# Attention, ELU layer and gated experts on one core: two large SBUF buffers are allocated after the small tensors instead of before them

## The reference

```python
q, k, v: [4, 8, 576, 64] float32        # window of 64 positions back
scores = q @ k.T / sqrt(64), masked to 0 <= i - j < 64
x = softmax(scores) @ v                 # reshaped to 2304 tokens x 512
h = x @ w_in                            # 512 -> 2048
x = where(h > 0, h, exp(min(h, 0)) - 1) @ w_out
P = exp(x @ w_gate - max)               # 2304 x 8, then 8 rounds of row and
for _ in range(8):                      # column normalisation
    P /= P.sum(1) + 1e-9; P /= P.sum(0) + 1e-9; P *= N / E
for e in range(8):                      # 512 -> 1024 -> 512 per expert
    out += P[:, e:e+1] * (relu(x @ w1[e]) @ w2[e])
```

## The kernel before

| tensor | start byte | size | start modulo 64 |
|---|---|---|---|
| `yacc` | 1,152 | 36,864 | 0 |
| `xs` | 38,016 | 24,576 | 0 |
| `w1t`, `w2t` | 62,592 and 91,264 | 28,672 each | 0 |
| `wraw` | 119,936 | 28,672 | 0 |
| `pb` | 148,608 | 9,216 | 0 |
| `scratch` | 157,824 | 67,584 | 0 |
| `ss` (over `scratch`) | 157,824 | 43,008 | 0 |
| `hb` (over `scratch`) | 200,832 | 24,576 | 0 |
| `ident`, `ones`, `wg` | 225,408; 225,920; 226,432 | 512 each | 0 |
| `adder` | 226,944 | 32 | 0 |
| `gate` | 226,976 | 576 | 32 |
| `token_max`, `all_max`, `gate_shift`, `row_sum` | 227,552 to 227,648 | 4, 4, 4, 72 | 32, 0, 32, 0 |
| `col_part`, `col_sum` | 227,744; 227,776 | 32 each | 32, 0 |
| `share` | 227,808 | 512 | 32 |
| `logit_parts` | 228,320 | 1,024 | 32 |

## Time and profile before

### The profile page before, as it was taken

One profiled execution on the slowest core, in us unless ns is written; L12 is line 12 of the kernel. 1 busy time (PEld: TensorE's weight loads), 2 busy tenths in 40 slices (PEclk: granted clock), 3 DMA queues, 4 the chain that ended last, 5 costly groups with the idle time before them and its releaser, 6 DMA issues.

```text
span 1897.3 us, 31366 instructions
## 1 busy us (share of the span) xinstructions
PE 1869.2 (99%) x11628; PEld 1834.2 (97%) x11628; DVE 1497.2 (79%) x1834; ACT 847.5 (45%) x1411; POOL 648.6 (34%) x513
## 2 busy tenths in 40 slices
PE   8989999999999999999999999999999999999998
PEld 6779999999999999999999999999999999999998
DVE  5767877878998888878778778787787787787877
ACT  6866655656664524333334243343333333432422
POOL 6733242333243343232332423332423324233220
PEclk9989999999999999999999999999999999999999
DMA  9974766663466666766666666667666666666654
GB/s 255 296 290 142 253 218 209 212 217 139 187 217 229 241 235 209 246 216 219 218 226 215 218 217 229 216 207 250 209 225 217 223 225 209 220 232 207 219 185 150
DMA packets 96653, 414.73 MB, mean 219 GB/s; under 512 B 9576, under 2 KB 10744, under 8 KB 96504
## 3 DMA queue, kind: packets, MB, share of 16 engines
q1 hardware_dynamic: 96504, 412.74, 63.5%
HBM read 374.88 MB, written 37.82 MB: 218 GB/s over the span
## 4 chain that ended last, share of the span: by engine, by line
PE 90%; DVE 4%; issue 2%; ACT 1%; POOL 1%; DMA 1%; SPq 0%; DVEq 0%; ACTq 0%; POOLq 0%
PE ps L1317 29%; PE ps L1312 29%; PE ps L1319 29%; PE ps L1276 1%; PE ps L1302 1%; PE ps L1292 1%; DVE hb L1052 1%; DVE xs L944 1%; DMA wraw<-moe_w_out_dram 1%; DVE yacc L1079 0%; DVE hb L1006 0%; DVE ss L978 0%; POOL scratch L566 0%; ACT pb L811 0%; ACT pb L816 0%
## 5 line engine op out<-in xcount | busy, mean ns | idle before, releaser
L799 ACT ACTIVATE ss<-hb 128x768 fp32r<-128x768 f32 x420 | 347.6, 843 | 595.3 <-DVE hb L1059 284.7
L1312 PE MATMUL ps<-xs,w1t 128*128 128x384 f32 x1680 | 564.3, 336 | 9.9 <-DMA xs<-x_store 2.7
L1312 PE MATMUL ps<-ss,w2t 128*128 128x384 f32 x1680 | 563.1, 335 | 3.1 <-DVE yacc L1079 3.1
L1317 PE MATMUL ps<-xs,w1t 128*128 128x384 f32 x1680 | 564.8, 336 | 0.0
L1319 PE MATMUL ps<-xs,w1t 128*128 128x384 f32 x1680 | 563.4, 335 | 0.0
L1317 PE MATMUL ps<-ss,w2t 128*128 128x384 f32 x1680 | 563.2, 335 | 0.0
L1319 PE MATMUL ps<-ss,w2t 128*128 128x384 f32 x1680 | 562.4, 335 | 0.0
L1079 DVE TENSOR_TENSOR yacc<-ps,yacc 128x768 f32<-128x768 f32 x396 | 377.8, 954 | 165.8 <-PE ps L1319 160.9
L978 DVE TENSOR_TENSOR ss<-hb,ss 128x768 fp32r<-128x768 f32 x420 | 400.5, 957 | 21.2 <-ACT ss L799 11.4
L595 POOL TENSOR_TENSOR w1t<-wraw,w1t 128x512 fp32r<-128x512 f32 x140 | 187.3, 1350 | 486.1 <-DVE ss L978 306.1
L595 POOL TENSOR_TENSOR w2t<-wraw,w2t 128x512 fp32r<-128x512 f32 x140 | 184.7, 1339 | 444.1 <-DVE hb L1001 226.9
(11 more groups left out here) (101 smaller groups left out, 1286.5 us busy)
## 6 DMA issues: line engine op xcount, KB each, us to landing
xs<-x_store SPq DMA_DIRECT2D x388, 768.0 KB, 4.3
wraw<-moe_w_dram SPq DMA_DIRECT2D x32, 1024.0 KB, 7.1
x_store<-xs SPq DMA_DIRECT2D x32, 768.0 KB, 3.6
pb<-p_store SPq DMA_DIRECT2D x24, 384.0 KB, 4.3
x_store<-w2t SPq DMA_DIRECT2D x10, 768.0 KB, 6.5
scratch<-q_dram SPq DMA_DIRECT2D x16, 288.0 KB, 5.3
scratch<-k_dram SPq DMA_DIRECT2D x16, 288.0 KB, 6.8
scratch<-v_dram SPq DMA_DIRECT2D x16, 288.0 KB, 7.8
```

Source lines behind the costliest of these rows:

```text
L799: nc.scalar.activation(ss[:, step, 0, :], hq(r, HOME[step]), ACT.Copy).then_inc(s_hi_done, 1)
L1312: nc.tensor.matmul(bank, w_parts[:, step, 0, cols], hi, start=step in FRESH and kt == 0, stop=False, skip_group_check=True)
L1317: nc.tensor.matmul(bank, w_parts[:, step, 0, cols], lo, start=False, stop=False, skip_group_check=True)
```

## The change

The block that allocates `scratch`, `ss` and `hb` is moved from before `ident` to after `logit_parts`. Nothing else differs: no instruction, wait, queue or tensor size.

```diff
         pb = sb("pb", [P, CHUNKS, CT])
-
-        SS = STEPS * 2 * QN
-        HB = 2 * 4 * QN
-        with nc.sbuf_tensor("scratch", [P, SS + HB], F32) as scratch_tensor:
-            scratch_space = scratch_tensor[:]
-        ss = sb("ss", [P, STEPS, 2, QN], F32R)
-        hb = sb("hb", [P, 2, 4, QN])
         ident = sb("ident", [P, P])
         ones = sb("ones", [P, P])
...
         p_turned = logit_parts[0:PT]
+
+        SS = STEPS * 2 * QN
+        HB = 2 * 4 * QN
+        with nc.sbuf_tensor("scratch", [P, SS + HB], F32) as scratch_tensor:
+            scratch_space = scratch_tensor[:]
+        ss = sb("ss", [P, STEPS, 2, QN], F32R)
+        hb = sb("hb", [P, 2, 4, QN])
```

## The result

The changed kernel is slower: median 1920.98 us (1918.61 to 1921.98, 4 runs) against 1897.83 us (1895.19 to 1899.97, 4 runs) before, ratio 1.012 with a 95% interval of 1.0103 to 1.0139. That is 23.15 us. The profiled execution took 1919.68 us.

A forecast was written before the change was run, and what follows sets the result against it. The prediction took TensorE's matmul rate as the bound. Its five prices, 0 + 0 + 0 + 0 + 0, left the profiled 1899.13 us, so it forecast 1899 us, range 1891 to 1908, with 0.78 for no change within 0.3%.

The forecast's parts named there:

- The bound: Whole kernel: TensorE's matmul rate, 10,080 x 0.173 = 1744 us of 1897; placement matters through that rate or lateness beyond cover.
- each ns on a matmul of the product down: Product down, L1312, L1317, L1319: each ns costs 5.04 us; 1.13 ns per matmul would exceed the 5.7 us no-change margin.
- Matmuls that read `ss`: Product down, 5,040 matmuls with ss at 32 modulo 64: price taken as 0, upper bound 36 us.
- The rival: Product down: moving reads of ss at 32 modulo 64 get dearer, with an extra 64-byte piece 1935 us; chance 0.07.
- VectorE, ScalarE and GpSimd at 32 modulo 64: Elementwise work and attention: at most 10 ns per VectorE instruction, 3 ns per ScalarE, GpSimd 0; all hidden, cost 0.
- The loads of attention: 64 q, k, v loads into scratch: taken as 0, upper 2.4 us; rival that they come late, 1905 us, chance 0.03.
- The granted clock from 110 to 155 us: Sign to check in the changed kernel's profile, from 110 to 155 us: the clock stays near 0.89.
- The estimate from the Trainium skill: Rows of q and k in scratch: 79 beats of 76 by the 256-byte rule, 4%, sum about 1 us longer.
- another phase at start-up: Rival, 110 to 155 us: other arrival times remove clock loss and a GpSimd wait, giving 1891.4 us; chance 0.09.

The follow-up runs named there:

- e2: Kernel before, with adder (32 bytes) allocated ahead of scratch, so scratch, ss and hb move by only 32 bytes; 1894.95 us.
- f4: Kernel before, with ident, ones, wg, share and logit_parts ahead of scratch, so ss and hb go up by 3,072 bytes; 1893.04 us.
- r2: The kernel with ss and hb 3,072 bytes up from the kernel before, timed in five rounds; 1895.82 us, ratio 0.9999.
- g1: Kernel before, with three 32-byte tensors ahead of w2t: w2t and ss 96 bytes later, xs and w1t stay; 1903.38 us.
- g2: Kernel before, with xs and ss moved by 96 bytes modulo 256 and both weights w1t and w2t by 0; 1924.58 us.
- f3: Kernel before, with all tensors 160 bytes lower, so their differences of place stay; 1900.91 us.
- e4: Kernel before, with adder between ss and hb: hb alone at 32 modulo 64, ss at 0; 1895.84 us.
- r1: Changed kernel, with adder, col_part and col_sum behind hb, so ss moves up 3,840 bytes instead of 3,936; 1895.66 us, ratio 0.9999.
- e1: Changed kernel, with adder (32 bytes) allocated behind hb, so ss and hb start at multiples of 64; 1902.78 us, ratio 1.0039.
- f1: Kernel before, with step s of ss 32 x s bytes later and all tensors 896 bytes lower; 1903.43 us.
- f2: Kernel before, with step s of ss 128 x s bytes later, 0 to 768; 1899.83 us.

## Why the prediction was wrong

**The bound was read rightly.** TensorE's rate of matmuls sets the time, and a change of placement moves it only through that rate. The statement that each ns on a matmul of the product down costs 5 us, and that it decides from 1.13 ns, holds: it became 3.2 ns (38.3 / 12).

**The step that failed** is the first price, "Matmuls that read `ss`": I took 0. Three things were wrong in it.

*The variable.* I described the move by its remainder modulo 64 (32) and by absolute places. What counts is the distance from the weights modulo 256 (96). Before, `xs`, `ss`, `w1t` and `w2t` are all level modulo 256, because each size between them is a multiple of 256; the small tensors, 3,936 bytes, are not. The table of places showed this, and I didn't ask which places have a relation that the change breaks.

*The evidence.* I set 0 because weight loads of `share` and `logit_parts` at 32 modulo 64 last 187 and 190 ns. In the changed kernel, where their places modulo 64 are the same, they last 188 and 190. A weight load's own length says nothing of a moving stream. And equal rates for `xs` and `ss` said nothing of a price, since both were at distance 0. No row of before had any other distance in the round's matmuls; the price was open, not 0, and its chance of 0.07 was too small for a resource with no idle time.

*What pays.* The rival counted 5,040 matmuls. The product up pays as well, 28.3 of the 66.7 ns, in its first seven matmuls. The rival had the direction right and its 36 us were an upper bound that held, but for a wrong reason: no piece of 64 bytes is involved, since at 32 modulo 64 alone (e2) the price is 6.7 ns. Without the first group of seven products up, before which there is no product down, 59 rounds pay it: 66.7 ns x 7 x 59 = 27.5 us.

**From 27 us to 23.** The medians differ by 23.15 us here. Against the 1895.92 us that the kernel before took in the 23 later executions the changed kernel is 25.1 us longer, so part of the gap may be the spread of the few executions here; that was not tested. In the profiled executions the span grows by 20.5 us. Between 110 and 250 us the kernel before ran at a mean granted clock of 0.95 and the changed one at 0.98; its row of that stretch, then that of the changed kernel:

```profile
110.00:250.00 140.00, 129.28 (x715) 127.70 (x714) 102.24 (x109) 85.46 (x117) 45.53 (x33) 0.95 0.61 215
```

```profile
110.00:250.00 140.00, 129.97 (x726) 128.16 (x725) 104.55 (x111) 87.02 (x119) 46.71 (x33) 0.98 0.62 220
```

Eleven matmuls more at 0.173 are 1.9 us, and the dearer rate hides about as much again in that stretch (140 us x 1.6% = 2.2, an estimate); from 540 to 600 us (clock 0.97 and 1.00, 328 and 335 matmuls) it is another 1.2 and 1.0. So some 6 of the 27 us are given back there in this pair of executions. The clock of these stretches isn't tied to placement: f4 and r2 are the same kernel, and had 0.99 and 0.98 from 110 to 250 us and 1.00 and 0.97 from 540 to 600. Why single executions differ there was not tested.

**The other steps.** VectorE, ScalarE and GpSimd at 32 modulo 64: right, even less than the 10 and 3 ns allowed. The loads of attention: right in the main, one wait of 0.3 us on k and the last group of attention's matmuls begins at 110.94 us (111.17 before). The granted clock from 110 to 155 us, which was to stay near 0.89, averaged 0.92. The estimate from the Trainium skill ("DMA: Bandwidth & Descriptors", How a descriptor splits into AXI transactions) of about 1 us can't be seen: with `scratch` at 224 modulo 256 the k load's median was 8.4 us in the changed kernel, 6.6 in g1, 7.7 in g2 and 10.4 in f3, with 128 it was 6.8 in the kernel before, 7.6 in e4, 8.0 in f4, 7.9 in r2 and 7.0 in r1. The ranges overlap, so no run shows the page's rule for these writes. The rival "another phase at start-up" is real in size: f3 and f4 differ by 8 us at the same rate, and the kernel before by itself spreads over 7. Nothing ties it to the change.

**What stays open.** That the price goes with the distance between moving operand and weights modulo 256 bytes, and that at 96 bytes it outlasts a switch by seven matmuls, is shown. Why is not shown. That TensorE's two reads, of the moving operand and of the weights, get in each other's way would fit a pattern that repeats to the nanosecond, but it is a guess. The order of the curve (16 dear, 32 cheap, 48 dear) isn't explained. The operands of attention's matmuls lie mostly in `scratch` and moved together, so they show nothing of it.

## What to carry to other kernels

Where TensorE has no idle time and runs matmuls like these (fp32r, 128 x 128 by 384, a weight load for each; no others were tried), the place of a moving operand against the weights loaded meanwhile is part of its rate: keep them level modulo 256 bytes, and put small tensors with odd sizes behind the large ones or fill them up. When a change moves memory only, list the differences of place between tensors that are read together, not their alignment alone, and treat a price with no row as unknown. And compare counts per stretch, not busy time: 500.00 of 500 us was 2,887 matmuls in one kernel and 2,841 in the other.

## What the runs showed of the hardware that I had not expected

- The interval of these matmuls (128 x 128 by 384, fp32r) is 173.3 ns at distance 0 and on average 176.7 at 96 bytes (g2, where single intervals reach 180). The sequence of intervals repeats in every steady round: 30 rounds of a run differ by at most 1 ns.
- A distance in one product is paid in the next: behind a product at 64 bytes, itself cheap at 2,075 ns, the product up takes 2,105 (e1, f1).
- The period is 256 bytes: 0, 256, 512 and 768 alike, 128, 384 and 640 alike (f2: 2,080 and 2,117 ns for 12 matmuls).
- `hb`, which only VectorE and ScalarE read and write, has no price at 32 bytes (e4: 2,887 matmuls in 500 us).
